# A convolution mix and two MLPs on one core: softmax of a chunk's weights one phase earlier, transposition of the mixed tokens one step later

## The reference

```python
w = np.exp(weight_gen - np.max(weight_gen, axis=-1, keepdims=True))
w = w / (np.sum(w, axis=-1, keepdims=True) + 1e-09)
x_unf = x_pad[:, idx, :].reshape(B, S, K, H, group)      # a token and its six predecessors
x = np.einsum('bshk,bskhg->bshg', w, x_unf).reshape(B * S, D)
h = x @ moe_w_in;  x = np.maximum(0.01 * h, h) @ moe_w_out
h = x @ moe2_w_in; out = np.where(h > 0, h, np.exp(np.minimum(h, 0)) - 1) @ moe2_w_out
```

## Time and profile before

| what | value |
|---|---|
| runs | 1236.48, 1238.52, 1239.02 us; median 1238.52 us |
| profiled execution | 1236.35 us, its span 1234.6 us |
| PE busy (matmul) | 1156.0 us, 94% |
| DVE, ACT, POOL busy | 828.8, 740.3, 486.8 us |
| chain that ended last | PE 86%, issue 5%, DVE 4%, POOL 4%, ACT 1%, DMA 1% |
| mean granted TensorE clock | 0.976 of full speed |

### The profile page before, as it was taken

One profiled execution on the slowest core, in us unless ns is written; L12 is line 12 of the kernel. 1 busy time (PEld: TensorE's weight loads), 2 busy tenths in 40 slices (PEclk: granted clock), 3 DMA queues, 4 the chain that ended last, 5 costly groups with the idle time before them and its releaser, 6 DMA issues.

```text
span 1234.6 us, 24425 instructions
## 1 busy us (share of the span) xinstructions
PE 1156.0 (94%) x9808; PEld 1007.4 (82%) x9808; DVE 828.8 (67%) x817; ACT 740.3 (60%) x846; POOL 486.8 (39%) x411
## 2 busy tenths in 40 slices
PE   7698998989989899898989989899898989989998
PEld 4576887878889888787878889899787878889986
DVE  6969775756757567575765757567575766756564
ACT  3455756656665565656656565565656656565674
POOL 5919054270824609054180723609145180730000
PEclk9999999999999899899999999899899999999999
DMA  6220112010120200212011120200202001110000
GB/s 173 65 84 27 62 40 63 25 57 16 38 61 25 74 13 25 61 34 65 25 40 34 38 61 25 70 14 28 61 25 74 25 21 52 38 25 27 14 27 27
DMA packets 44651, 54.39 MB, mean 44 GB/s; under 512 B 4116, under 2 KB 32914, under 8 KB 44624
## 3 DMA queue, kind: packets, MB, share of 16 engines
q1 hardware_dynamic: 44624, 54.01, 14.5%
HBM read 36.29 MB, written 17.69 MB: 44 GB/s over the span
## 4 chain that ended last, share of the span: by engine, by line
PE 86%; issue 5%; DVE 4%; POOL 4%; ACT 1%; DMA 1%; SPq 0%; POOLq 0%
PE y_a_rows L617 27%; PE hidden L549 27%; PE y_b L610 19%; PE hidden L553 9%; PE hidden L578 4%; DVE hid_lo L1116 1%; POOL mix L323 1%; POOL prod L311 1%; PE hidden L579 1%; DVE act L1086 1%; DMA xw<-in_x_dram 1%; DVE up_b_lo L998 0%; DVE act L1089 0%; POOL prod L336 0%; DVE up_a_lo L988 0%
## 5 line engine op out<-in xcount | busy, mean ns | idle before, releaser
L617 PE MATMUL y_a_rows<-hid_hi,dn 64*128 64x512 f32 x2048 | 577.0, 394 | 0.0
L1116 DVE TENSOR_TENSOR hid_lo<-act,hid_hi 128x1024 fp32r<-128x1024 f32 x255 | 338.5, 1328 | 217.0 <-ACT hid_hi L908 217.0
L610 PE MATMUL y_b<-hid_hi,dn 64*128 64x512 f32 x1024 | 403.3, 394 | 50.4 <-issue 46.5
L610 PE MATMUL y_b<-hid_lo,dn 64*128 64x512 f32 x1024 | 400.3, 391 | 0.0
L617 PEld LDWEIGHTS y_a_rows<-hid_hi,dn 64*128 64x128 f32 x2048 | 339.8, 188 | 26.6
L617 PE MATMUL y_a_rows<-hid_lo,dn 64*128 64x512 f32 x1024 | 355.8, 392 | 0.0
L908 ACT ACTIVATE hid_hi<-act 128x1024 fp32r<-128x1024 f32 x255 | 268.3, 1052 | 1.7 <-DVE act L1089 1.5
L311 POOL TENSOR_TENSOR mix<-xw,wk 128x384 f32<-128x384 f32 x30 | 27.1, 904 | 579.9 <-DVE wk L1026 577.0
L893 ACT ACTIVATE act<-hidden 128x1024 f32<-128x1024 f32 x127 | 130.5, 1027 | 204.4 <-PE hidden L553 162.5
L610 PEld LDWEIGHTS y_b<-hid_hi,dn 64*128 64x128 f32 x1024 | 192.1, 188 | 72.5 <-issue 54.3
L311 POOL TENSOR_TENSOR prod<-xw,wk 128x384 f32<-128x384 f32 x180 | 243.3, 1358 | 9.4
(11 more groups left out here) (105 smaller groups left out, 1109.5 us busy)
## 6 DMA issues: line engine op xcount, KB each, us to landing
xw<-in_x_dram SPq DMA_DIRECT2D x14, 960.0 KB
raw_b<-squares_out SPq DMA_DIRECT2D x60, 96.0 KB, 2.2
out_dram<-staged SPq DMA_DIRECT2D x15, 384.0 KB, 2.3
squares_in<-prod SPq DMA_DIRECT2D x56, 96.0 KB, 4.5
squares_out<-ya SPq DMA_DIRECT2D x15, 256.0 KB, 2.0
raw_a<-squares_in SPq DMA_DIRECT2D x14, 256.0 KB, 2.9
raw_d<-in_moe_w_out_dram SPq DMA_DIRECT2D x8, 384.0 KB, 4.2
raw_a<-in_moe_w_in_dram SPq DMA_DIRECT2D x8, 256.0 KB, 4.1
```

The source lines that it names most:

```text
L610: return nc.tensor.matmul(y_b[:, :], dn[m][rows, f, P:2 * P], v[rows, s % HB, HALF[i]], start=start, stop=stop)
L617: return nc.tensor.matmul(bank[:, :], dn[m][rows, f, first:first + P], v[rows, s % HB, HALF[i]], start=(f == 0 and n == 0), stop=(f == FT ...
L1116: nc.vector.tensor_tensor(hid_lo[:, s % HB, :], act[:, s % 2, :], hid_hi[:, s % HB, :].bitcast(f32), ALU.subtract).then_inc(s_lo, 1)
```

## The change

Softmax of chunk c+3 is done in the ELU phase of chunk c, which is one phase earlier than before: `softmax_a` in step 3, `softmax_exp` in step 4, `softmax_b` in step 5. Chunk 2 keeps its old place. `turn_mix` moves from step 1 to step 2, behind `add_y`, and the two input parts move from steps 4 and 5 to steps 5 and 6. One more pair of phases is written out behind the loop. At the start `load_chunk(2)` is issued ahead of `load_up(1, 2)`.

```diff
-            with eng.Fori(2, CH - 1) as c:
+            with eng.Fori(2, CH - 2) as c:
                 emit(0, c, phase_mlp1(c), 1, c - 2)
                 emit(1, c - 1, phase_mlp2(c - 1), 0, c)
+            emit(0, CH - 2, phase_mlp1(CH - 2), 1, CH - 4)
+            emit(1, CH - 3, phase_mlp2(CH - 3), 0, CH - 2)
...
-            load_up(1, 2)
...
             load_chunk(2)
+            load_up(1, 2)
             load_up(1, 3)
...
-                    if m == 1 and s in (4, 5) and not (known(c) and c >= CH - 2):
-                        mlp1_input_hi(c + 2, s - 4)
+                    if m == 1 and s in (5, 6) and not (known(c) and c >= CH - 2):
+                        mlp1_input_hi(c + 2, s - 5)
...
-                    if m == 0 and s == 1 and not (known(c) and c in (0, CH - 1)):
-                        softmax_exp(c + 1)
+                    if m == 0 and s == 1 and known(c) and c == 1:
+                        softmax_exp(2)
+                    if m == 1 and s == 4 and not (known(c) and c >= CH - 3):
+                        softmax_exp(c + 3)
...
-                    if m == 0 and s == 0 and not (known(c) and c in (0, CH - 1)):
-                        softmax_a(c + 1)
-                    if m == 0 and s == 2 and not (known(c) and c in (0, CH - 1)):
-                        softmax_b(c + 1)
-                    if m == 1 and s == 1 and not (known(c) and c >= CH - 2):
+                    if m == 0 and s == 0 and known(c) and c == 1:
+                        softmax_a(2)
+                    if m == 0 and s == 2 and known(c) and c == 1:
+                        softmax_b(2)
+                    if m == 1 and s == 2 and not (known(c) and c >= CH - 2):
                         turn_mix(c + 2)
-                    if m == 1 and s in (4, 5) and not (known(c) and c >= CH - 2):
-                        mlp1_input_lo(c + 2, s - 4)
+                    if m == 1 and s in (5, 6) and not (known(c) and c >= CH - 2):
+                        mlp1_input_lo(c + 2, s - 5)
+                    if m == 1 and s == 3 and not (known(c) and c >= CH - 3):
+                        softmax_a(c + 3)
+                    if m == 1 and s == 5 and not (known(c) and c >= CH - 3):
+                        softmax_b(c + 3)
```

## The result

The changed kernel takes 1179.86 us (median of 4 runs, 1179.55 to 1180.68), the kernel before 1237.50 (median of 4). The ratio is 0.9535, 95% interval 0.9519 to 0.9552. The profiled execution took 1180.68 us against 1236.35, so it is 55.7 us shorter; the forecast was 55.4.

A forecast was written before the change was run, and what follows sets the result against it. Bound: TensorE stalls because VectorE awaits GpSimd's late mix signal in turn_mix, ahead of yb. Terms: -46.5 - 19.2 + 4.4 + 5.9 = -55.4 us, from 1236.35 to 1181.0; with 2.2 for the median 1183.1, stated 1182, range 1173 to 1197.

The forecast's parts named there:

- The stalls: TensorE's 13 waits of 3.6 us ahead of a down product in the ELU phase would go: gain 46.5 us.
- The half-rate spells: Slow-clock stretches of TensorE behind the 3.6 us waits in the loop would go: 1.5 us each, 19.2 in all.
- Clock 1.00 from 124 us: Sign expected in the changed profile: TensorE at clock 1.00 from 124 us to near the end.
- The tail of step 2: ELU phase: TensorE waits in step 4 for VectorE's nonlinearity of step 2, hidden until now; 13 x 0.34 = +4.4 us.
- Moves at no cost: turn_mix, softmax_a and softmax_exp fit idle gaps on VectorE and ScalarE: cost nothing, 0.1 us of cover left behind turn_mix.
- The seam: Start of the leaky phase: input subtraction, slowed to 1242 ns beside GpSimd, delays TensorE 0.45 us, 13 times: +5.9 us.
- the 13 waits of 0.45 us at the matmul: Sign expected: TensorE waits about 13 times some 0.45 us for in_b at a leaky phase's first up product.
- The 9 us for all chunks: Cost at the leaky phase's start if the subtraction waits for one whole GpSimd product: 0.7 us each, 9 in all.
- The way through DRAM: Later turn_mix, result wanted by ScalarE one step later: taken as zero; other bound 0.8 us each, 10 in all.
- The rest: One pair of phases written out and two loads exchanged at the start: zero, give or take 1 us.
- the slower case: ELU step 3: softmax_a waits for late weights, holding up TensorE; at 6 us per chunk 1261 us, chance 0.03.
- shorter waits suffice: Rival for TensorE's clock: the slow clock stays because shorter waits are enough to bring it; 1201 us, chance 0.05.

The follow-up runs named there:

- kernel 5: The kernel before with turn_mix three instructions later, directly behind add_y in step 2; softmax and input parts unmoved: 1203.41 us, ratio 0.9727.
- kernels 1 and 3: Each against the kernel before. 1: turn_mix to step 2, input parts to steps 5 and 6: 1185.16 us. 3: softmax_b from step 2 to 1: 1175.79 us.
- the third job: The changed kernel run again, unaltered, in its third job on the chip: 1181.16 us, ratio 0.9539 to the kernel before.
- kernel 7: As kernel 4, with the copy of ylow out of PSUM moved from ScalarE to VectorE: 1173.44 us, ratio 0.9480.
- kernel 4: The changed kernel with softmax_b moved from step 5 to step 6, behind the subtraction for in_b: 1177.46 us, ratio 0.9520.
- kernels 6 and 7: 6: changed kernel with turn_mix in step 1, input parts in steps 4 and 5, ylow copied by VectorE: 1173.89, again 1172.75 us; 7: see kernel 7.

## Why the prediction was right

The mechanism was the forecast one: the stalls went with the late signal, the slow clock went with the stalls, and two smaller waits came up in step 4 and at the seam. By its parts, for 13 chunks each:

1. **The stalls, -46.5.** Right: no such wait is left. That the queue position ahead of `yb` carried them is shown by kernel 5, and that a lead of only 3.6 us was missing by kernels 1 and 3. "A whole phase earlier" gives 23.6 us of room, of which the kernel needs next to nothing.
2. **The half-rate spells, -19.2.** Right: the clock is 1.00 through the loop. Kernel 5 adds that they thin out with shorter stalls rather than vanish at once. "Clock 1.00 from 124 us" did not hold in each execution: the third job shows 0.64 from 124 to 128 us, behind a wait of 2.04 us.
3. **The tail of step 2, +4.4.** 0.34 was taken from two undisturbed phases; 0.43 each was measured, 5.6. The reason given, `take_y` on ScalarE, is borne out in part: kernel 7, with one of its two copies gone, has 0.57 us in place of 0.86 at the weight load of step 4.
4. **Moves at no cost.** 0.24 us of cover was left behind `turn_mix`, where I had 0.1, and TensorE did not wait.
5. **The seam, +5.9.** 0.40 each was measured (69.62 against 70.02), 5.2 in all. The size was nearly right by luck, by two errors that offset each other. I took the subtraction at 1242 ns and it took 939, since only the rest of one GpSimd product stood in its way. And I held that without GpSimd TensorE would not wait, which is wrong: kernel 4 still pays 0.16. I had compared the input's end with the first matmul at 148.25; the weight load ahead of that matmul waits for it first, 0.2 us earlier, as the kernel before shows:

```profile
148.03 0.19 PEld L549 LDWEIGHTS hidden<-in_a_hi,up_a_hi 64*128 64x128 f32 x2
```

So the wait showed as gaps of the weight loads, and not as the 13 waits of 0.45 us at the matmul that I had named as a sign. The rule of the Trainium skill (SBUF — State Buffer, "SBUF: two separate sides"), that the later one is held until the other's instruction is over, agrees with the timeline in kind: the product that begins at 357.22 would last until 358.09 alone, 0.40 us beyond the 357.69 of the subtraction, which was lengthened by 0.25. Why it is 0.15 less is not shown. The 9 us for all chunks, for a whole product in the way, were not reached.
6. **The way through DRAM, 0.** Right: no wait of ScalarE for the `raw_a` of the squares is left. With the large load out of the way, the squares land in 2.0 us instead of 4.5. In kernel 1 the load goes out 2.5 us ahead of them; they land in 2.3 us, and ScalarE does not wait. In kernel 5 it goes out 0.6 us ahead, as in the kernel before; they land in 4.6 us, and ScalarE waits in 10 chunks; there the transposition is later too, while the input parts kept their steps. So the bound was generous for the changed kernel, but a wait of this kind is near when the load goes out just ahead of the squares.
7. **The rest, 0.** The parts with their measured sizes make -46.5 - 19.2 + 5.6 + 5.2 = -54.9, against -55.7 measured. Between the matmuls of the earlier trace rows, 130.89 and 1166.20 before, 131.00 and 1110.98 after, it is 55.3 us, so 0.4 stays open there. Another 0.7 us came from the very end, where TensorE turns the last output. The kernel before does this from 1229.09 at 1.2 GHz for the most part (0.50 from 1230 to 1232), the changed kernel from 1173.84 at 2.4 GHz (1.00 from 1172.8 to 1174.8; duration ns min/median/max):

```profile
L726 PE MATMUL hidden<-ident,ya x4: 328/450/472, 1229.1 to 1230.9; 128*128 128x128 f32 x4
```

```profile
L728 PE MATMUL hidden<-ident,ya x4: 327/328/331, 1173.8 to 1175.2; 128*128 128x128 f32 x4
```

No part of the forecast had this.

Of the rivals, none came up in the changed kernel's loop. In the slower case `softmax_a` would have waited for its weights; they were asked for 20.8 us ahead, and it does not wait.

What the forecast did not see is that its two halves were not worth the same. Kernel 2 (softmax early alone) gives 1175.3, kernel 1 (transposition alone) 1185.2, the whole 1179.4. The fastest found are kernels 6 and 7, 1172.75 and 1173.44 us on one chip, with overlapping intervals and pairs of 69.48 and 69.52; that is some 8 us below the changed kernel beside them (1181.16).

## What to carry to other kernels

An engine's wait is paid by whatever stands behind it in its queue: ask first what that is and whether it could stand ahead, and how late the signal is, before moving a whole stage. A lateness of 3.6 us was cured by one step for one function, while moving a consumer nearer to its deadline put new waits where none had been. And when a stall goes, the chains it had covered come up; they can be read in advance in the phases that never had the stall.

## What the runs showed of the hardware

- A stall of TensorE costs more than its length through the clock, but not each time. At 3.58 us nine of twelve intervals between stalls lost 1.6 to 2.5 us more to spells at 1.2 GHz; at 2.07 us (kernel 5) three of twelve lost 1.5. The wait of 2.0 us ahead of the loop brought a spell in one of three profiled executions of the changed kernel. The forecast had held it unlikely (0.05) that shorter waits suffice; at 2 us they did at times, while 0.43 to 0.99 us brought none in the loops of these kernels.
- A VectorE subtraction with both inputs in SBUF takes 685 ns alone and 939 or 1242 ns beside GpSimd, which fits a wait for what is left of GpSimd's instruction; GpSimd's first product takes 1.74 us in place of 0.87 when it comes second.
- The idle time ahead of a matmul understates how late its input is: 0.43 us on PE went with 0.86 us on the weight loads, and 0.51 us there with nothing listed on PE.
- A small write right behind a large load of the same queue lands later. The four writes of the squares (96 KB each) took 4.5 and 4.6 us to land 0.6 us behind the load of 960 KB (kernel before, kernel 5), 2.3 us when 2.5 us behind it (kernels 1 and 3), and 2.0 us with no load near (changed kernel). The rows of kernels 5 and 1:

```profile
squares_in<-prod SPq DMA_DIRECT2D x56, 96.0 KB, 4.6
```

```profile
squares_in<-prod SPq DMA_DIRECT2D x56, 96.0 KB, 2.3
```
